# VectorE's attention work split around the gate, and six suffix scans joined into one, in a fused attention and MLP kernel

## The reference, cut to what matters

```python
def _attn_ref(r, k, v, w, u):               # B, H, S, D = 4, 8, 768, 48
    for t in range(S):
        cur = np.einsum('bhd,bhe->bhde', u[None] * kt, vt)
        y[:, :, t] = np.einsum('bhd,bhde->bhe', rt, state + cur)
        state = wt[:, :, :, None] * state + np.einsum('bhd,bhe->bhde', kt, vt)

def _moe_ref(x, w_in, w_out):               # 3072 tokens, 384 -> 2048 -> 384
    h = x @ w_in
    return ((h * np.cos(h)) @ w_out).astype(np.float32)

def _moe2_ref(x, phi, w1, w2):              # 8 experts with 4 slots each
    logits = x @ phi
    ...
    return (c @ slot_out).astype(np.float32)
```

## Time and profile before

| what | us |
|---|---|
| three runs, median | 724.79 |
| lowest, highest | 723.89, 725.16 |
| the profiled execution | 725.35 |
| its span | 723.5 |
| TensorE busy in it | 603.3 |
| VectorE busy | 508.8 |
| ScalarE busy | 320.6 |
| GpSimd busy | 221.0 |

### The profile page before, as it was taken

The page is one execution under the profiler, slowest core; times in us unless marked ns, Lnnn a source line. Parts: engine busy times, 40 slices in busy tenths (PEclk is TensorE's granted clock), DMA queues, the critical chain, the costliest instruction groups (busy, mean ns, idle before and its releaser), DMA issues.

```text
span 723.5 us, 12474 instructions
## 1 busy us (share of the span) xinstructions
PE 603.3 (83%) x4549; PEld 527.8 (73%) x4549; DVE 508.8 (70%) x1297; ACT 320.6 (44%) x693; POOL 221.0 (31%) x193
## 2 busy tenths in 40 slices
PE   0534799979998999899989998899979899985892
PEld 0423788969887888788878888788879889972242
DVE  5793889488949794889578967987698854542413
ACT  1522344544464536453644474446534546452012
POOL 4451233244224332432242423342334223220000
PEclk9965999999999999999999999999999999996897
DMA  9941304310422041214021313112310019863336
GB/s 294 341 152 43 110 3 153 103 53 2 154 80 74 2 153 29 87 40 154 8 98 50 101 55 103 50 57 99 105 49 18 2 44 415 343 213 136 128 134 262
DMA packets 44295, 81.39 MB, mean 112 GB/s; under 512 B 4160, under 2 KB 26816, under 8 KB 44224
## 3 DMA queue, kind: packets, MB, share of 16 engines
q1 hardware_dynamic: 44224, 80.48, 32.4%
HBM read 71.02 MB, written 4.72 MB: 105 GB/s over the span
## 4 chain that ended last, share of the span: by engine, by line
PE 58%; DVE 23%; ACT 8%; issue 6%; POOL 2%; DMA 1%; SPq 1%; DVEq 0%; ACTq 0%; POOLq 0%
PE yb L773 20%; PE hb L760 18%; DVE zs L942 4%; PE ab L686 4%; PE ab L705 3%; PE ab L711 3%; DVE ang L1090 3%; DVE r_end L978 2%; DVE ang L1098 2%; DVE A L989 2%; PE ab L724 2%; PE pb L783 2%; PE yb L887 1%; DVE tmp L956 1%; ACT turns L572 1%
## 5 line engine op out<-in xcount | busy, mean ns | idle before, releaser
L489 POOL TENSOR_TENSOR g_lo<-ang,g_hi 128x384 fp32r<-128x384 f32 x128 | 129.4, 1011 | 403.0 <-DVE g_hi L1103 403.0
L760 PE MATMUL hb<-x_hi,win 128*128 128x384 f32 x768 | 219.5, 340 | 26.3 <-DVE ang L1098 19.6
L773 PE MATMUL yb<-wout,g_hi 128*128 128x384 f32 x768 | 206.1, 349 | 2.4 <-POOL g_lo L489 2.4
L760 PEld LDWEIGHTS hb<-x_hi,win 128*128 128x128 f32 x768 | 141.6, 189 | 33.8 <-DVE ang L1098 26.6
L773 PEld LDWEIGHTS yb<-wout,g_hi 128*128 128x128 f32 x768 | 133.3, 189 | 14.1 <-issue 7.2
L578 ACT ACTIVATE ang<-ang 128x384 f32<-128x384 f32 x128 | 67.2, 525 | 164.7 <-DVE ang L1090 164.6
L773 PE MATMUL yb<-wout,g_lo 128*128 128x384 f32 x384 | 129.2, 336 | 0.0
L760 PE MATMUL hb<-x_lo,win 128*128 128x384 f32 x384 | 129.1, 336 | 0.0
L572 ACT ACTIVATE turns<-hb 128x384 int32<-128x384 f32 x128 | 62.8, 491 | 117.4 <-PE hb L760 117.4
L1090 DVE SCALAR_TENSOR_TENSOR ang<-turns,hb 128x384 f32<-128x384 int32 x128 | 70.6, 552 | 61.9 <-ACT turns L572 61.2
L1098 DVE SCALAR_TENSOR_TENSOR ang<-ang,hb 128x384 f32<-128x384 f32 x128 | 69.8, 546 | 46.6 <-ACT ang L580 46.6
(11 more groups left out here) (157 smaller groups left out, 684.1 us busy)
## 6 DMA issues: line engine op xcount, KB each, us to landing
over_att<-w_dram SPq DMA_DIRECT2D x8, 1536.0 KB, 12.5
zs<-zs_dram SPq DMA_DIRECT2D x16, 384.0 KB, 3.4
zp<-zp_dram SPq DMA_DIRECT2D x16, 384.0 KB, 3.8
kT<-k_by_channel_dram SPq DMA_DIRECT2D x16, 384.0 KB, 5.0
rT<-r_by_channel_dram SPq DMA_DIRECT2D x16, 384.0 KB, 6.0
over_win<-w_dram SPq DMA_DIRECT2D x4, 1536.0 KB, 8.9
over_wout<-w_dram SPq DMA_DIRECT2D x4, 1536.0 KB, 6.7
r_tok<-r_by_token_dram SPq DMA_DIRECT2D x16, 288.0 KB, 5.1
```

What stands on the lines that cost most here:

```text
L489: g.tensor_tensor(g_lo[f % RING][:, :], ang[f % 2][:, :], g_hi[f % RING][:, :].bitcast(F32), ALU.subtract).then_inc(glo_done, 1)
L760: last = t.matmul(hb[f % 2][:, 0:TT], win[:, f, w, k, :], x[:, k, :], start=(n == 0), stop=(n == 3 * DK - 1))
L773: last = t.matmul(yb[c][:, 0:DM], gx[f % RING][:, c * P:(c + 1) * P], wout[:, f, w, :], start=(f == 0 and n == 0), stop=(f == NF - 1 and n ...
```

## The change

VectorE's function `attention` becomes two. `attention_first` is called where `attention` was, between angle and gate; `attention_second` is called behind gate and cast, ahead of post. Ahead are now the two maxima (step 0), the flags, `tmp` and the first line of `sigma` (step 1), the four blocks of `A` (step 2), the multiplication of `r_end` and the verdict (step 3), the scaling of the first state (step 5), the last state and the general path (step 6). Behind are the suffix scan, `ptot` and `fine` (step 0), the rest of `sigma`, `seed` and `diag` (step 1), `vsum` and the scan `r_end` (step 2), the eight blocks of `A` (step 3), the predicated copies (steps 4 and 5) and two states (step 5). The maximum over `zp` moves from step 1 to step 0, and the four blocks of step 2 stand ahead of `vsum` and the scan. The six scans become one of 768 elements, with ones in `ends` at each 128th column, where the scan starts anew; `ends` grows from 128 to 768 columns. Nothing changes on the other engines.

```diff
-                    for m in range(CHUNKS):
-                        part = zs[q][:, m * P:(m + 1) * P][:, ::-1]
-                        last = v.tensor_tensor_scan(part, part, ends[:, ::-1], 0.0, ALU.mult, ALU.add)
-                    last.then_inc(suffix_done, 1)
...
+            def attention_second(T, q, step, own):
+                if step == 0:
+                    wait(dve, chain, T, NCHAIN, own[0])
+                    v.tensor_tensor_scan(zs[q][:, ::-1], zs[q][:, ::-1], ends[:, ::-1], 0.0, ALU.mult, ALU.add).then_inc(suffix_done, 1)
...
                     if att is not None:
                         for q in range(QUADS):
-                            attention(att, q, slot - QUAD_SLOT[q], own)
+                            attention_first(att, q, slot - QUAD_SLOT[q], own)
                     if mid is not None:
                         gate(mid, slot)
+                    if att is not None:
+                        for q in range(QUADS):
+                            attention_second(att, q, slot - QUAD_SLOT[q], own)
                     if late is not None:
                         post(late, slot - POST_SLOT, own_post)
```

More of the change, by code:

```diff
@@ L929, in nth, with attention_first @@
                 return 1
-            def attention(T, q, step, own):
+            def attention_first(T, q, step, own):
                 if step == 0:
@@ L960, in attention @@
                     v.tensor_scalar(sg[:, :], fine[:, :], -1.0, 1.0, ALU.mult, ALU.add).then_inc(chain, nth(own))
+                if step == 2:
+                    diagonal_blocks(T, q, (0,))
+                if step == 3:
+                    wait(dve, kr_in[q], T, 32, 32)
+                    wait(dve, chain, T, NCHAIN, own[0])
+                    v.tensor_tensor(r_end[:, :], rT[q][:, :], r_end[:, :], ALU.mult).then_inc(ends_done, 1)
+                    was_read(dve, T, use_of(q, "flag"))
+                    v.tensor_copy(verdict[q][:, :], vsum[:, :]).then_inc(verdict_done, 1)
@@ new lines, in attention_first @@
+                if step == 5:
+                    if not isinstance(T, int) or T:
+                        was_read(dve, T - 1, use_of(q, "a2h1"))
+                    st = state[:, q, 0, :, :]
+                    v.tensor_scalar(st, st, keep[:, 0:1], None, ALU.mult).then_inc(state_done, 1)
+                if step == 6:
+                    next_state(T, q, 2)
+                    wait_apart(dve, (chain, T, NCHAIN, own[0]))
+                    general_path(T, q)
+                    dve.sem_inc(a_done, 1)
@@ new lines, in diagonal_blocks @@
+            def diagonal_blocks(T, q, cs):
+                if cs[0] == 0:
+                    if q:
+                        y_made(dve, T, 0)
+                    elif not isinstance(T, int) or T:
+                        y_made(dve, T - 1, 1)
+                wait(dve, diag_done, T, QUADS, q + 1)
+                for c in cs:
+                    for h in range(4):
+                        v.tensor_scalar(A[:, h % 2, c, h // 2, :], ident[:, :], diag[:, c, h:h + 1], None, ALU.mult).then_inc(spread, 1)
@@ new lines, in next_state @@
+            def next_state(T, q, c):
+                if c < CH - 1:
+                    wait(dve, state_done, T, QUADS * 2, q * 2 + c + 1)
+                else:
+                    was_read(dve, T, use_of(q, "a2h0"))
+                    wait(dve, scaled_done, T, QUADS * CH * PAIRS, q * CH * PAIRS + PAIRS)
+                side, col = KV_AT[c]
+                b = bank_of(use_of(q, f"a2h{side}"))
+                for pp in range(PAIRS):
+                    last = v.scalar_tensor_tensor(state[:, q, (c + 1) % CH, pp, :], state[:, q, c, pp, :],
+                                                  ptot[:, pp * CH + c:pp * CH + c + 1],
+                                                  ab[b][:, col + pp * D:col + (pp + 1) * D], ALU.mult, ALU.add)
+                last.then_inc(ab_read[b] if c else state_done, 1)
@@ new lines, in attention_second @@
+            def attention_second(T, q, step, own):
+                if step == 0:
+                    wait(dve, chain, T, NCHAIN, own[0])
+                    v.tensor_tensor_scan(zs[q][:, ::-1], zs[q][:, ::-1], ends[:, ::-1], 0.0, ALU.mult, ALU.add).then_inc(suffix_done, 1)
+                    wait(dve, suffix_done, T, QUADS, q + 1)
+                    v.tensor_tensor(ptot[:, :], zp[q][:, 1::P], zs[q][:, ::P], ALU.mult).then_inc(chain, nth(own))
+                    wait(dve, chain, T, NCHAIN, own[0])
+                    v.tensor_scalar(fine[:, :], ptot[:, :], P_LEAST, None, ALU.is_ge).then_inc(chain, nth(own))
+                if step == 1:
+                    sg = sigma[q]
@@ L979, in attention @@
                 if step == 3:
[L980 to L989, removed]
+                    diagonal_blocks(T, q, (1, 2))
                 if step in (4, 5):
@@ L1005, in attention @@
                             masked.then_inc(chain, nth(own))
[L1006 to L1031, removed]
+                if step == 5:
+                    next_state(T, q, 0)
+                    next_state(T, q, 1)
             def general_path(T, q):
```

15 lines of the change are left out of this document (3 added, 12 removed).

## The result

The changed kernel took 773.38 us (median of four runs, 771.67 to 774.67), the kernel before 724.83; the ratio is 1.067 with a 95% interval of 1.065 to 1.069. The prediction was 769.0 us (730 to 782), slower with 0.83.

The account below looks back on a forecast made before the run. VectorE's queue in slots 0 to 4 and TensorE elsewhere were taken as bounds in turn. +39 us in six tiles, +5.5 in the first and -0.2 in the prologue gave +44.3, so 769 us, range 730 to 782.

Parts of the forecast that it names:

- Two bounds that take turns: VectorE's queue bounds slots 0 to 4, TensorE the rest, with 1.15 us of TensorE slack where they meet.
- 2.56 us plus the piece: Each VectorE slot with a long piece behind the gate takes 2.56 us plus that piece.
- Port waits in slot 0: Slot 0 of quad 0: g_lo(0) waits for the scan, fine for k_end (1.82 us); slot 7.05 us, +1.9.
- The A blocks: Slot 3: eight blocks of 1.57 us meet g_lo(3), 0 to 1.0 us of waiting, 0.5 taken; 4.65 us, difference +0.3.
- The sum by stretches of a pass: Pass +6.5 us: +2.6 by slot 6, +0.6 in slot 8, +1.5 in slots 9 and 10, +1.8 in slot 11.
- The last term: Slot 11: scaled waits for next_state behind gate, cast and copies, so lT's exponential reaches TensorE later, +1.8 us.
- Six passes, the first, the prologue: Six full tiles +39 us, the first of seven +5.5, the prologue -0.2, the last tile 0; sum +44.3.
- The clock: Rival, chance 0.07: idle at flags and exp lowers TensorE's clock on two groups a tile, 23 us more, 792 us.
- The other two rivals: No new port wait, 732 us, chance 0.14; faster, hb's gate waits of 19.6 us all go, 706 us, chance 0.13.

Follow-up runs that it names:

- first version with everything ahead: The kernel before with the joined scan, all ahead of the gate, and maximum over zp, tmp, diag and lT's copy moved: 724.78 us, ratio 0.9996.

## Why the prediction was right

**Two bounds that take turns**. Confirmed: the copies alone (37 us) and the rest alone (8 us) do not add up to the 53 of both, since TensorE's slack at the copies is used once.

**2.56 us plus the piece.** Confirmed to 0.2 us in each of slots 1 and 2 and to 0.02 in slot 4 (table above). The 0.2 of slot 2 go with the low clock behind the flags: with matmuls in that idle time the slot took 4.29 us.

**Port waits in slot 0**. Confirmed by row (`fine` 1.73, g_lo(0) 2.38) and by the run that let k_end wait: `fine` fell to 0.17. I had 7.05 us, it was 6.84; g_lo(0) got the port 0.2 us before the scan's recorded end, so that ptot took 0.79 us where I had looked for over 1, and k_end followed without a gap. What the prediction did not say is how little this is worth: with the copies ahead of the gate, port waits and all cost 0.8 us a pass. It is the copies behind the gate that turn them into time. What the port waits alone are worth there no run shows, since the one that took `fine`'s away lost the gain to the clock.

**The A blocks.** 2.44 us, 0.8 above the 1.64 of the earlier trace rows: GpSimd got in between, nearer to the 1.0 than to the 0.5 that I took. Slot 3 was 4.92 for 4.65.

**The sum by stretches of a pass.** From the angles' starts: by slot 6 the pass is late by 2.8 us (summed: 2.6), by slot 9 by 3.1 (3.2), by slot 11 by 4.6 (4.7), by slot 12 by 6.9 (6.5). The last term was mis-sized: 2.3 us for 1.8. cast(11) waits there 0.98 us for yb(9), as cast(5) did in quad 0, where I had counted it; the copies and with them next_state and scaled come that much later:

```profile
374.36 0.36 DVE L1113 CAST g_hi<-ang 128x384 fp32r<-128x384 f32 x1 [0.98 <-PE yb L773]
```

**Six passes, the first, the prologue.** The six took 41.6 us more (39 summed), the first 6.8 (5.5), the last 0.2, and what follows it 0.8 less, for which I had nothing. The first pass started 1.4 us earlier, where I had 0.2; why stays open: the kernel with the joined scan alone, whose maximum over `zp` has not moved, started as early, and the one with the copies alone behind the gate, which has the same scan, only 0.3 us earlier. Together that is 46.4 us between the spans of the two profiled executions (723.5 and 769.9), where I had 44.3. The profiled one, 771.67 us, is the fastest of the four, so that the medians lie 48.6 apart.

**The clock**, a rival with 0.07 at +23 us, was there and was not: it falls behind the flags in each pass, which I had given a price, and costs 0.14 us a pass since VectorE is the bound. Its full price shows only in the traces of kernels next to this one. The other three executions of the changed kernel were 1.5 to 3.0 us longer than the profiled one, at granted clocks of 0.938, 0.934 and 0.929 against 0.947, so it may have cost them that; they have no trace. The other two rivals are out: `fine` did wait, and VectorE's five slots took 23.5 us, not 17.5.

## What to carry to other kernels

Moving long pieces behind a wait takes idle time off one consumer and gives it to all others: ask of each moved instruction who reads it next and how much slack that reader has; here the copies and states had 1.15 us and were moved by 2.1. When two engines share a port, a stalled instruction that is moved away hands its wait to the next of its kind; place them where the other engine's queue cannot yet be at it. And put the saving of one stretch against the engine that bounds the next one, before adding up waits.

## What the runs showed of the hardware

- VectorE instructions of six elements and GpSimd's k_end do not overlap: `fine` went from 1.73 to 0.17 us when k_end was moved, and tmp (1.08 in the kernel before) and sigma (1.76 in the first version with everything ahead) waited for it in the same way. A reduction (the maximum over `zp`, 0.92 to 0.95 us) and the flags' steps (0.15 each) run beside GpSimd at full speed. By the Trainium skill's SBUF — State Buffer, section Who interferes with whom, a VectorE instruction with two SBUF inputs or in a two-port mode and a GpSimd instruction exclude each other, and whichever starts later stands still. The traces agree in both directions: g_lo took 2.38 to 2.46 us, for 1.02, when a scan of 1.75 had started 0.16 earlier.
- A waiting GpSimd instruction gets in at the next boundary between two VectorE instructions: behind one scan of 768 elements (ptot 1.19), between eight short blocks (2.44 for 1.64). One row of the prologue is against it: r_tok's product took 4.12 us for 1.4 and did not get in between two VectorE subtractions of 1.74. What decides stays open.
- Idle time of TensorE of 1.6 to 3.4 us can be followed by the low level of its clock (granted 0.50) for 3 to 6 us, and need not be: the same 2.64 us was followed by it in all six full passes of one kernel, in three of another, and in none of the changed one. 14 matmuls that nothing reads, put into that idle time, kept the clock up and made a kernel 10.6 us faster. What decides stays open; no run here takes it apart.
